# Attention stage of a fused kernel: row turns on VectorE, heads paired h and h+4, residents loaded behind the inputs

## The reference

```python
# 1. retention ("attention"), per batch and head, gamma_h = 1 - 2**(-5-h)
for t in range(768):
    state = gamma * state + outer(k[t], v[t])
    y[t] = q[t] @ state / 8
x = y laid out as (3072 tokens, 512)
# 2. routing by logits = x @ w_gate, greedy over all pairs by falling logit, 8 experts, 384 tokens each
#    expert e:  h = relu(x[mask] @ w1[e]);  out[mask] = h @ w2[e]       (512 -> 1024 -> 512)
# 3. GLU:  (sigmoid(x @ w_gate2) * (x @ w_val)) @ w_out                (512 -> 1536 -> 512)
```

## Time and profile before

| what | value |
|---|---|
| median of 3 runs | 1093.22 us |
| profiled execution, its own time | 1091.62 us |
| its span | 1089.5 us |
| mean granted clock of TensorE | 0.979 |
| PE busy | 1032.4 us (95%) |
| DVE busy | 674.9 us (62%) |
| ACT busy | 346.2 us (32%) |
| POOL busy | 130.5 us (12%) |
| PE busy in tenths, 40 slices of 27.2 us | 6999943999999999999999999999999999999996 |
| granted clock in the same slices | 9999965999999999999999999999999999999998 |

### The profile page before, as it was taken

One profiled execution on the slowest core, in us unless ns is written; L12 is line 12 of the kernel. 1 busy time (PEld: TensorE's weight loads), 2 busy tenths in 40 slices (PEclk: granted clock), 3 DMA queues, 4 the chain that ended last, 5 costly groups with the idle time before them and its releaser, 6 DMA issues.

```text
span 1089.5 us, 20139 instructions
## 1 busy us (share of the span) xinstructions
PE 1032.4 (95%) x7256; PEld 962.4 (88%) x7256; DVE 674.9 (62%) x1825; ACT 346.2 (32%) x659; POOL 130.5 (12%) x157
## 2 busy tenths in 40 slices
PE   6999943999999999999999999999999999999996
PEld 5888822999999999999999999999999999999995
DVE  3665468877577657756776677656775677554211
ACT  3444433422333223322332233223412341224110
POOL 5543401033010101010100010011001100110001
PEclk9999965999999999999999999999999999999998
DMA  9999543313341324123321332142314231324000
GB/s 201 248 243 238 136 136 107 117 40 87 78 131 55 87 78 126 59 77 88 108 78 58 108 98 87 47 119 88 97 40 126 75 110 34 116 78 122 1 1 29
DMA packets 186986, 107.67 MB, mean 99 GB/s; under 512 B 80784, under 2 KB 169360, under 8 KB 186896
## 3 DMA queue, kind: packets, MB, share of 16 engines
q1 hardware_dynamic: 183056, 93.94, 32.7%
q0 software_dynamic: 3840, 12.59, 3.6%
HBM read 88.41 MB, written 18.09 MB: 98 GB/s over the span
## 4 chain that ended last, share of the span: by engine, by line
PE 94%; DVE 3%; DMA 1%; issue 1%; SPq 0%; POOL 0%; ACT 0%; DVEq 0%; POOLq 0%
PE bank L1277 21%; PE bank L1279 20%; PE bank L1278 20%; PE bank L1370 6%; PE bank L1371 6%; PE bank L1369 6%; PE bank L663 2%; PE bank L640 2%; PE bank L636 2%; PE bank L597 1%; PE bank L1237 1%; PE bank L604 1%; PE bank L615 1%; PE bank L650 1%; PE bank L621 1%
## 5 line engine op out<-in xcount | busy, mean ns | idle before, releaser
L1277 PE MATMUL bank<-h2h,resident 128*128 128x384 f32 x768 | 261.6, 341 | 0.0
L1279 PE MATMUL bank<-h2h,resident 128*128 128x384 f32 x768 | 258.2, 336 | 0.0
L1278 PE MATMUL bank<-h2l,resident 128*128 128x384 f32 x768 | 257.6, 335 | 0.0
L1277 PEld LDWEIGHTS bank<-h2h,resident 128*128 128x128 f32 x768 | 144.4, 188 | 3.2
L1278 PEld LDWEIGHTS bank<-h2l,resident 128*128 128x128 f32 x768 | 144.4, 188 | 2.9
L1279 PEld LDWEIGHTS bank<-h2h,resident 128*128 128x128 f32 x768 | 144.2, 188 | 0.0
L804 ACT ACTIVATE ring<-ring_raw 128x512 fp32r<-128x512 f32 x192 | 117.6, 623 | 61.5 <-DMA ring_raw<-in_moe_w_out_dram 42.0
L1110 DVE TENSOR_TENSOR pf<-bank,gate 128x384 f32<-128x384 f32 x96 | 53.5, 557 | 128.2 <-PE bank L1279 120.4
L828 ACT ACTIVATE ph<-pf 128x384 fp32r<-128x384 f32 x96 | 50.4, 525 | 252.7 <-DVE pf L1110 242.7
L1119 DVE TENSOR_TENSOR ring<-ring_raw,ring 128x512 fp32r<-128x512 f32 x192 | 126.2, 684 | 0.0
L824 ACT ACTIVATE gate<-bank 128x384 f32<-128x384 f32 x96 | 46.9, 489 | 147.1 <-PE bank L1279 147.0
(11 more groups left out here) (187 smaller groups left out, 1668.4 us busy)
## 6 DMA issues: line engine op xcount, KB each, us to landing
ring_raw<-in_moe_w_dram SPq DMA_DIRECT2D x128, 256.0 KB, 3.1
ring_raw<-in_moe_w_out_dram SPq DMA_DIRECT2D x64, 256.0 KB, 2.8
qraw<-in_q_dram SPq DMA_DIRECT2D x24, 256.0 KB, 4.4
kraw<-in_k_dram SPq DMA_DIRECT2D x24, 256.0 KB, 5.1
vraw<-in_v_dram SPq DMA_DIRECT2D x24, 256.0 KB, 5.2
xrows<-xrow SPq DMA_DIRECT2D x24, 256.0 KB, 3.6
xlaid<-xg SPq DMA_DIRECT2D x7, 768.0 KB, 4.5
zg<-xlaid SPq DMA_DIRECT2D x28, 192.0 KB, 4.6
```

The costliest lines, as they stand in the source:

```text
L1277: nc.tensor.matmul(ps, wh, xhi, start=start, stop=False)
L1278: nc.tensor.matmul(ps, wh, xlo, start=False, stop=False)
L1279: return nc.tensor.matmul(ps, wl, xhi, start=False, stop=stop)
```

## The change

- The x^T to rows turn leaves TensorE: xT is written by VectorE (two multiplications of the products with a table `growth`, which takes the place of the q scaling and of SCALE), and a VectorE transpose in 32x32 blocks makes rows of it. The x rows then lie in blocks in SBUF, and a store is four DMAs of 32 partitions each, in 512-byte pieces, instead of one.
- q goes unscaled to TensorE. `growth` is made once at the start, by 24 transposes of the spread decay table in slot 1, copied by ScalarE.
- Heads are paired h and h+4 instead of 2a and 2a+1. The raw q and k tiles interleave them, so each load of q and of k is two DMAs. The state is kept as 64x64 per head, in one addition over 128 partitions; state products contract over 64 rows into 64 partitions, four and then four value products, twice a unit. Key-value products are paired in the same way.
- On TensorE, scores stand ahead of the transposes. On VectorE the order is logits, masks, transpose, growth, state.
- The loads of q and k are issued as soon as their buffer is free, v later in the slot.
- All residents are loaded behind the inputs: four groups of four in SyncE's last slots, the rest after them, the last seven (SHARED, four before) behind the last store. All 28 high halves are made on ScalarE after the attention, all low halves on GpSimd behind the first gather: the first eight at once, the next eight one behind each h product, the other 12 as before.

```diff
-        EARLY_EACH = 4
-        EARLY = EARLY_EACH * B
-        LATE_EACH = 4
+        EARLY = 16
+        GROUPED = 4
         LATE = RESIDENT - EARLY
+        SHARED = 7
...
+                def load(raw, src, u, landed):
+                    b, c = divmod(u, C)
+                    for r in range(2):
+                        sp.dma_start(raw[:, c, r:H:2, :],
+                                     src[b, r * (H // 2):(r + 1) * (H // 2), c * P:(c + 1) * P, :]
+                                     .rearrange("h s d -> s h d")).then_inc(landed[c], 16)
...
+                def store(u):
+                    c = u % C
                     sp.wait_ge(xrow_ready, u + 1)
+                    for j in range(QUADS):
+                        sp.dma_start(xrows[u * P:(u + 1) * P, j * P:(j + 1) * P].rearrange("(t i) x -> i t x", i=QUAD),
+                                     xrow[j * QUAD:(j + 1) * QUAD, c, :].rearrange("i (t x) -> i t x", x=P)).then_inc(xrow_stored[c], 16)
...
+                group = 0
+                for s in range(U + 4):
+                    if 0 <= s - 1 < U - C:
+                        sp.wait_ge(qk_transposed, 2 * (s - 1) + 1)
+                        load(qraw, q, s - 1 + C, q_loaded)
+                        sp.wait_ge(ks_ready, s)
+                        load(kraw, k, s - 1 + C, k_loaded)
+                    if 0 <= s - 3 < U - C:
...
+                        load_v(s - 3 + C)
+                    if 0 <= s - 4 < U:
+                        store(s - 4)
+                    if s >= U - C + 3 and group < EARLY // GROUPED:
+                        for r in range(group * GROUPED, (group + 1) * GROUPED):
+                            load_resident(sp, r)
+                        group += 1
...
-                def split_early(n, k):
-                    r = EARLY_EACH * n + k
...
-                    nc.gpsimd.tensor_copy(resident[:, r, 0, :], resident_raw[r][:, :]).then_inc(resident_hi, 1)
-                    pool.wait_ge(resident_hi, r + 1)
-                    resident_low(r)
...
+                def grow():
+                    for c in range(C):
+                        act.wait_ge(spread_turned, c + 1)
+                        nc.scalar.activation(growth[:, c, :, :], ps_y[c % 2][:, :].rearrange("p (a t) -> p a t", a=KD),
+                                             ACT.Copy, scale=SCALE).then_inc(growth_ready, 1)
...
-                        nc.vector.tensor_tensor(qs[:, c % 2, :, :], qraw[:, c, :, :],
-                                                dec[:, 0, c, :].unsqueeze(2).to_broadcast([P, H, D]),
-                                                ALU.mult).then_inc(qs_ready, 1)
...
+                        nc.vector.transpose(xrow[:, cc, :].rearrange("p (t j a) -> p a t j", j=QUAD, a=KD),
+                                            xTa[:, cc % 2, :, :].rearrange("p a (t i) -> p a t i", i=QUAD)).then_inc(xrow_ready, 1)
...
+                        for n in range(2):
+                            nc.vector.tensor_tensor(xTa[:, cc % 2, 2 * n:2 * n + 2, :], ps_y[n][:, 0:2 * P].rearrange("p (a t) -> p a t", a=2),
+                                                    growth[:, cc, 2 * n:2 * n + 2, :], ALU.mult).then_inc(xT_ready, 1)
...
-                        for a in range(KD):
-                            last = nc.tensor.transpose(ps_x[:, a:DM:KD],
-                                                       xTa[:, cc % 2, a, :], ident[:, :])
-                        last.then_inc(x_transposed, 1)
...
+                        for pair in range(2):
+                            heads = [r * NPAIR + 2 * pair + n for r in range(2) for n in range(2)]
+                            def place(h):
+                                return ps_y[h // NPAIR][h % 2 * D:h % 2 * D + D, pair * P:(pair + 1) * P]
                             if cc > 0:
+                                for h in heads:
+                                    r, a = divmod(h, NPAIR)
+                                    rows = slice(r * D, r * D + D)
+                                    nc.tensor.matmul(place(h), state[rows, cc % 2, a, :], qT[rows, cc % 3, a, :],
                                                      start=True, stop=False)
+                            for h in heads:
+                                last = nc.tensor.matmul(place(h), vraw[:, cc, h, :], att[:, cc % 2, h, :], start=cc == 0, stop=True)
...
-            for k in range(LATE):
-                pool.wait_ge(val_done if k % 2 else gate_done, k // 2 + 1)
-                late_low(k)
+            for r in range(RESIDENT):
+                if r >= EARLY:
+                    pool.wait_ge(val_done if r % 2 else gate_done, (r - EARLY) // 2 + 1)
+                elif r >= KF:
+                    pool.wait_ge(h_done, r - KF + 1)
+                low(r)
...
+            for r in range(RESIDENT):
+                high(r)
```

More of the change, by code:

```diff
@@ L359, in attend_sync @@
             def attend_sync(sp):
[L360 to L368, removed]
+                sp.dma_start(dec[:, :, :, :], decay).then_inc(dec_loaded, 16)
@@ L379, in attend_sync @@
-                for b in range(B - 1):
-                    for c in range(C):
-                        store(b, c)
+                        sp.dma_start(wr[:, :, 0:E], w_router.rearrange("(t p) e -> p t e", p=P)).then_inc(wr_loaded, 16)
+                group = 0
[6 more added lines that the diff above has]
+                    if 0 <= s - 3 < U - C:
+                        b, c = divmod(s - 3, C)
@@ L383, in attend_sync @@
                         if c < C - 1:
                             sp.wait_ge(kv_done, b * (C - 1) + c + 1)
-                        load(b + 1, c)
-                        if c >= C - EARLY_EACH:
-                            load_resident(sp, EARLY_EACH * (b + 1) + c - C + EARLY_EACH, early_loaded[b + 1])
-                for c in range(C):
-                    store(B - 1, c)
+                        else:
+                            sp.wait_ge(y_done, s - 2)
+                        load_v(s - 3 + C)
@@ L578, in attend_tensor, with turn_spread @@
                 pe.wait_ge(consts_ready, 4)
-                pe.wait_ge(tables_loaded, 32)
-                pe.wait_ge(state_cleared, 1)
-                pe.wait_ge(pick_made, 1 + KD)
+                def turn_spread():
+                    for c in range(C):
+                        pe.wait_ge(spread_ready, c + 1)
+                        if c >= 2:
+                            pe.wait_ge(growth_ready, c - 1)
+                        for a in range(KD):
+                            last = nc.tensor.transpose(ps_y[c % 2][:, a * P:(a + 1) * P], spread[:, c % 2, a * P:(a + 1) * P], ident[:, :])
+                        last.then_inc(spread_turned, 1)
                 def body(b, c, s):
@@ L587, in body @@
                         pe.wait_ge(parts_ready, u + 1)
+                        if s == 5:
+                            pe.wait_ge(pick_made, 1 + KD)
                         nc.tensor.matmul(ps_l[:, 0:E], lparts[:, cc % 2, :], pick[:, :], start=True, stop=True).then_inc(logits_done, 1)
+                    if alive(s, 2):
+                        bb, cc = unit(b, c, 2)
+                        u = bb * C + cc
+                        pe.wait_ge(kT_ready, u + 1)
+                        if s is None or s - 2 >= 1:
+                            pe.wait_ge(att_ready, 2 * u)
+                        for a in range(NPAIR):
+                            for r in range(2):
+                                rows = slice(r * D, r * D + D)
+                                last = nc.tensor.matmul(ps_s[r][:, a * P:(a + 1) * P], kT[rows, cc % 2, a, :],
+                                                        qT[rows, cc % 3, a, :], start=True, stop=True)
+                                if a == NPAIR - 1:
+                                    last.then_inc(scores_done, 1)
                     if alive(s, 1):
```

225 lines of the change are left out of this document (103 added, 122 removed).

## The result

| | us |
|---|---|
| before, 6 runs | 1093.16 (1091.51 to 1094.58) |
| after, 6 runs | 1098.11 (1095.95 to 1098.59) |
| ratio | 1.004, 95% interval 1.003 to 1.0051 |
| span of the profiled execution | 1089.5 before, 1096.9 after |

The change makes the kernel slower by 0.4%. The forecast was 1085 in a range of 1074 to 1092, with 0.85 on faster: wrong in sign, and the time lies outside the range.

The account below looks back on a forecast made before the run. TensorE's work was taken to bound the attention. Attention -17.6, low halves +8.3 and +1.0 make -8.3 us: 1083.3 from the profiled execution, 1085 for the median, against 1093.2 before; range 1074 to 1092.

Parts of the forecast that it names:

- What bounds the kernel: In the attention TensorE's own work is the bound; the DMA engines, nearly full there, are next.
- Attention, slots 5 to 24: TensorE's slot in the attention falls from 5.49 to 4.86 us, saving 12.6 us.
- full overlap and 0.10 a change, 0.74: State products in a TensorE slot: four at once, 0.10 us per change of form, 0.74 instead of 0.88.
- Is something else late: At a 4.86 us slot, VectorE's 3.84 is hidden and DMA issue at 4.6 a unit is charged nothing.
- Head: Time before slot 5: TensorE starts sooner but gains 24 growth-table transposes; -2.5 us, bounds 0 and -4.
- Tail: From slot 24 to the last logits, 17.5 us becomes 15.0: -2.5 us, bounds 0 and -4.
- Low halves of the first eight: Behind the third gather, VectorE and GpSimd take turns, making the first x low 8.3 us late; bounds nothing and 9.
- my list of seven: VectorE operations behind the third gather (two L909, L915, four L1119), each expected to wait 1.29 us for GpSimd.
- The other eight ... I take +1: Low halves one per h tile, where VectorE feeds TensorE with little to spare: +1 us, bounds 0 to 4.
- Sum: Whole kernel: attention -17.6, low halves +8.3 and +1.0, together -8.3 us.
- The sign of being wrong: The forecast is wrong if the attention ends later than 135 us; last logits were expected at about 126.
- rival 3: Attention slot: only pairs of products overlap, each change of form costs 0.15; slot 5.45, 1097 us, slower; chance 0.12.

Follow-up runs that it names:

- e3: Changed kernel with products ordered value pair 0, states 0, states 1, value pair 1, one change of matmul form less a slot; 1093.50 us, ratio 1.0003 to the kernel before.
- e1: Changed kernel with 16 early residents loaded one a slot by SyncE and split on GpSimd in the attention; 1091.84 us, ratio 0.9982 to the kernel before.
- e10: e9 with the 24 growth-table turns put ahead of the first q transposes; 1082.85 us, ratio 0.9899 to the kernel before.
- e9: e7 with the product order of e3; 1083.15 us, ratio 0.9905 to the kernel before.
- e11: Changed kernel with GpSimd's first low half held until VectorE's conversion of the digits is done; 1092.31 us, one run.
- e12: Changed kernel with VectorE's first four ring pieces (low halves of the first weight pieces) put ahead of the conversion of the digits; 1095.97 us, one run.
- e7: e1 with the residents' loads issued by ScalarE instead of SyncE, ScalarE's slots written out one by one; 1083.23 us, one run.
- e5: Changed kernel with the conversion of the digits made a tensor_tensor addition of ones instead of a tensor_scalar; 1098.26 us, one run.
- e6: e3 with scores put last on TensorE and masks last on VectorE, as in the kernel before; 1102.04 us, one run.
- e2: Changed kernel with GpSimd's first eight low halves held until the four x lows are made; 1093.33 us, ratio 0.9999 to the kernel before.

## Why the prediction was wrong, by its own steps

In the span the forecast was 15.7 us too low (-8.3 against +7.4): 5.7 in the slots of the attention, where the changes of matmul form were mis-sized; 2.5 in the head; 6.5 between the first expert matmul and the first gate product, most of it TensorE's clock, which had no term; and 1.0 in the tail and ahead of the first expert matmul together.

- **What bounds the kernel**: right. TensorE sets the slots, and it still does after the change.
- **Attention, slots 5 to 24**: forecast a slot of 4.86 and 12.6 us, got 5.19 and 6.9. The x transposes gave their 0.44. State products were taken at "full overlap and 0.10 a change, 0.74"; the overlap was real (0.44 instead of 0.88), but 1.94 - 0.44 - 0.88 leaves 0.62 for four changes of form against 0.15 for the one before, so that the part came to 0.03 more instead of 0.14 less. That is the term that failed. A change costs 0.15 to 0.17 (here and in e3), the upper bound of 0.15 that I read from one group or a little more, and I had taken 0.10. The rest, 0.15: the q transposes cost 0.10 more behind the scores, which I had not priced, and the gap of 0.05 for the logits copy was not there to win: the earlier trace rows shows none. By the Trainium skill, "TensorEngine Tiling (Array Packing)", section Key Properties, a change of tiling mode drains TensorE; e3 agrees, with 0.17 us here.
- **Is something else late**: VectorE's terms came as worked out (transpose 1.13 against 1.11, growth 0.42 against 0.38). SyncE was put at 4.6 us a unit; it is 4.96 in the middle, so the margin to TensorE is 0.2. It did not bite in the changed kernel, and did in e1.
- **Head**: forecast -2.5, got 0. TensorE began 3.4 us earlier (4.94 against 8.36), but the 24 turns then held it from 8.06 to 13.66, and the first scores came at 13.66 against 13.93. I had priced the turns at 0.27 each and still expected a gain. e10 moved them ahead, and slot 5 began 2.3 us earlier than in e9.
- **Tail**: forecast -2.5, got -2.3.
- **Low halves of the first eight**: forecast +8.3, got +9.13 before the first expert matmul. The size was near, the mechanism wrong: not seven operations that each wait 1.29, but one that waits eight times. Turn-taking as I described it would have cost about 6 (e11: 48.97 against 42.8 to 43.5 with no low halves), since the x lows' PSUM input spared them and later ring pieces stood behind them. So the near size is luck, and so is the sign that I named for it, 13.5 us from the third gather's issue to the first x low, which came out at 14.4. The Trainium skill's "SBUF — State Buffer", Who interferes with whom, says that the shared ports are held by one of the two at a time, and that the order of issue decides which one blocks; here VectorE's had started 0.3 us first, and it was the one that waited, through eight instructions of the other (e12). The measurement decides.

  The trace of the kernel before held the operation that matters, and my list of seven began just behind it: the third gather ends at 181.80, and VectorE then had this one in progress.

```profile
181.52 0.35 DVE L967 TENSOR_SCALAR digit_f<-digit_i 128x168 bf16<-128x168 int32 x1
```

- **"The other eight ... I take +1"**: to gate got 7.50 longer, the largest miss of one term. The low halves beside the h tiles are 3.2 of it: I had read that VectorE feeds TensorE "with little to spare" there and bounded it at 4, so they lie inside the bounds and above the +1. The other 4.3 are the clock, for which the sum had no term. Where no low halves stand there (e1, e7, e9, e10) to gate is still 38.84 to 39.78 against 37.28, because the first passes run at the 1.2 GHz level. This part may be no loss of the change: the profiled execution of the kernel before had a mean granted clock of 0.979, but 45 of the 48 executions behind its medians beside the experiments had 0.974 to 0.977, and no trace of one of those was kept. The rest, a longer stretch at the lower level and the second fall, goes with a mean clock of 0.969 (here and in e5; 0.972 to 0.974 in e3, e6 and e12, which lack the fall), and five of the changed kernel's six executions have 0.969. So most of them probably had it; that is inferred from the mean clock, and what brings it on stays open.
- **Sum**: attention -9.2 instead of -17.6 (8.4 off), all behind it +16.6 instead of +9.3 (7.3 off). Forecast -8.3, measured +7.4 in the span and +4.95 in the medians. The sign of being wrong, an attention that ends later than 135, was set too wide: it ended at 134.6, with 8.4 of the 17.6 us missing.
- **Rivals**: the slower side was given to the slot alone (rival 3, 0.12), and the low halves to one value. The slot came out about midway between the forecast and rival 3 (5.19 between 4.86 and 5.45), and behind the first expert matmul it was more than the upper end of 4. I had summed each at its middle, and the range had no room for the two together. No rival had the clock.

## What to carry to other kernels

Splitting work that one engine has time for, at a stage where it is idle, is worth a look at the queue that feeds it: moving 16 DMA issues from SyncE to ScalarE (e1 to e7) was worth 8.6 us (one run of e7) with no byte moved more or less. Work moved out of a stage in which another engine is the bound must be priced where it lands; here it landed twice on VectorE's path, and moving it within that path (e2) only moved the loss. When a change splits one form of matmul into two that alternate, count the changes of form first, and order the products so that like stands by like.

## What the runs showed of the hardware

- A VectorE instruction in progress when a run of GpSimd subtractions began 0.30 to 0.31 us later lasted as long as the run: 10.24, 10.32 and 10.675 us beside eight, 5.35 beside four, for a tensor_scalar and for tensor_tensor alike. With 0.17 us between the starts (e2) the VectorE instruction took its usual 0.68, and there, as when the two began together (e11), they alternated from then on (a ring piece's 0.68 becomes 1.74 to 1.76, a low half's 1.23 becomes 1.42 to 1.55).
- A change of matmul form between 128-row, 64-column products and 64-row, 64-column products costs 0.15 to 0.17 us; four 64x64 products run at once (0.22 us for eight records of 128 columns).
- In the middle of the changed kernel's attention SyncE issues a DMA in 0.51 to 0.57 us, be it 64, 128 or 256 KB; nine a unit are 4.96 us. With a tenth (e1) the stores took 0.70 each and the unit 6.1. It is not a constant: in the kernel before a load of 256 KB took 0.43 to 2.2 us to issue.
- The granted clock at the first expert matmul was at the upper level in the profiled execution of the kernel before (passes 0.17 us apart from 187.03) and at the lower for 3.4 us in e7, though TensorE did the same just ahead: twelve transposes in 2.83 us and a wait of 0.62. It cost 1.6 us in e7. Executions of the same code differ too: behind the same wait of 2.5 us the clock fell in the changed kernel and in e5, and did not in e3, e6 and e12. What decides it stays open.
